# Reordering the steps between the last expert of layer one and the first tiles of layer two, on four engines, with one more wait for the weight loads

## The reference, cut to what matters

```python
x = attention(q, k, v)                       # 1536 x 512
# layer one: 8 experts, each token goes to the best 2 of its noisy scores
out[mask] += top2_w[mask, k, None] * (relu(x[mask] @ w1[e]) @ w2[e])
# layer two: other weights, each token goes to its best expert alone
logits = x @ w_gate + modality_bias[modality_id]
e_idx  = argmax(logits, axis=1)
out[mask] = gate_w[mask, None] * (relu(x[mask] @ w1[e]) @ w2[e])
```

## Time and profile before

| | us |
|---|---|
| median of 3 runs | 673.99 (672.82 to 674.08) |
| the profiled execution: its time | 674.08 |
| the profiled execution: its span | 672.0 |
| PE busy in the span | 639.0 |

### The profile page before, as it was taken

The page is one execution under the profiler, slowest core; times in us unless marked ns, Lnnn a source line. Parts: engine busy times, 40 slices in busy tenths (PEclk is TensorE's granted clock), DMA queues, the critical chain, the costliest instruction groups (busy, mean ns, idle before and its releaser), DMA issues.

```text
span 672.0 us, 11238 instructions
## 1 busy us (share of the span) xinstructions
PE 639.0 (95%) x3866; PEld 580.1 (86%) x3867; DVE 329.8 (49%) x681; ACT 275.7 (41%) x529; POOL 184.7 (27%) x199
## 2 busy tenths in 40 slices
PE   7989999899999999999999999999988999999981
PEld 6989999898999999999999999988767888788871
DVE  4466645588365526254361634467876222542220
ACT  5667866442344335252443523144516123522110
POOL 2500100117362533516144251201652121121010
PEclk9999999999999999999999999999998999999996
DMA  7867822263684646646355520724649211001000
GB/s 209 281 235 240 291 74 80 66 249 74 237 214 138 132 148 157 190 142 156 111 122 177 148 28 3 171 63 159 171 138 387 102 48 47 20 32 48 16 32 11
DMA packets 51089, 89.84 MB, mean 134 GB/s; under 512 B 7919, under 2 KB 14063, under 8 KB 51040
## 3 DMA queue, kind: packets, MB, share of 16 engines
q1 hardware_dynamic: 41872, 69.21, 31.0%
q0 software_dynamic: 9168, 19.97, 13.3%
HBM read 73.13 MB, written 17.02 MB: 134 GB/s over the span
## 4 chain that ended last, share of the span: by engine, by line
PE 82%; DVE 6%; DMA 3%; ACT 3%; issue 2%; SPq 1%; ACTq 0%; POOL 0%; DVEq 0%; POOLq 0%
PE banks L1060 6%; PE banks L1059 6%; PE banks L999 6%; PE banks L1078 6%; PE banks L1001 6%; PE banks L998 6%; PE banks L803 5%; PE banks L831 4%; PE banks L1377 3%; PE banks L1342 3%; PE banks L1347 3%; PE banks L1343 3%; PE banks L1373 3%; PE banks L1374 3%; PE banks L815 2%
## 5 line engine op out<-in xcount | busy, mean ns | idle before, releaser
L1833 DVE TENSOR_TENSOR split<-stage,split 128x2048 fp32r<-128x2048 f32 x32 | 73.3, 2290 | 41.9 <-ACT split L1463 41.8
L998 PE MATMUL banks<-xTs,split 128*128 128x416 f32 (+1 forms) x256 | 88.6, 350 | 0.0
L999 PE MATMUL banks<-xTs,split 128*128 128x416 f32 (+1 forms) x256 | 86.5, 342 | 0.0
L650 POOL DMA_INDIRECT x_moe<-rows,dst_idx x25 | 49.3, 1971 | 113.2 <-DVE rows L2285 112.2
L1059 PE MATMUL banks<-hTs,split 128*128 128x416 f32 x224 | 79.9, 357 | 0.0
L1060 PE MATMUL banks<-hTs,split 128*128 128x416 f32 x224 | 78.6, 351 | 0.0
L1598 ACT ACTIVATE hTs<-banks 128x416 fp32r<-128x416 f32 x56 | 29.0, 518 | 81.6 <-PE banks L1001 81.6
L1463 ACT ACTIVATE split<-stage 128x2048 fp32r<-128x2048 f32 x32 | 60.9, 1908 | 1.0 <-DMA stage<-w1a 1.0
L1720 ACT ACTIVATE hTs<-banks 128x512 fp32r<-128x512 f32 x28 | 16.5, 596 | 105.8 <-PE banks L1357 105.8
L1001 PE MATMUL banks<-xTs,split 128*128 128x416 f32 (+1 forms) x256 | 56.2, 340 | 0.0
L803 PE MATMUL banks<-k_sb,q_sb 128*128 128x260 f32 (+2 forms) x192 | 49.6, 384 | 3.5 <-DMA k_sb<-k_w 2.1
(11 more groups left out here) (371 smaller groups left out, 1308.3 us busy)
## 6 DMA issues: line engine op xcount, KB each, us to landing
stage<-w1a SPq DMA_DIRECT2D x16, 1024.0 KB, 7.6
stage<-w2a SPq DMA_DIRECT2D x16, 1024.0 KB, 5.4
k_sb<-k_w SPq DMA_DIRECT2D x12, 520.0 KB, 5.0
raw<-w1b SPq DMA_DIRECT2D x4, 1024.0 KB, 7.9
raw<-w2b SPq DMA_DIRECT2D x4, 1024.0 KB, 9.7
q_sb<-q_t SPq DMA_DIRECT2D x24, 128.0 KB, 3.1
x_attention<-rows SPq DMA_DIRECT2D x12, 256.0 KB, 6.1
split<-x_moe SPq DMA_DIRECT2D x12, 256.0 KB, 3.6
```

The costliest lines, as they stand in the source:

```text
L650: pool.indirect_dma_start(out=x_dram[1], out_offset=rows_at(dst_idx[0], early_dst, e, k), in_=y_lines(e, k), in_offset=None, compute_op=AL ...
L998: pe.matmul(psum, piece(slot, 0, o + c * FH), xTs[:, 0, c, 0:cols], start=(c == 0), stop=False)
L999: pe.matmul(psum, piece(slot, 1, o + c * FH), xTs[:, 0, c, 0:cols], start=False, stop=False)
L1833: dve.tensor_tensor(split_chunk(e % 2, 1, c), staged_chunk(e % 2, c), split_chunk(e % 2, 0, c).bitcast(F32), ALU.subtract).then_inc(low_do ...
```

## The change

It reorders steps on PE, ACT and DVE and adds one wait on SP.

- SP: before it loads the second expert of layer two, it also waits until the gather of tile 2 has landed (`gathered[0]` at 32).
- PE: `back(last, 3)` moves ahead of `first(0, 0)`; `ranks(1)` and a wait for all four scaled parts of the last expert move ahead of `first(0, 1)`; `codes2` moves out of `second(0)` to a place behind `first(1, 1)`. Tile 3 becomes an ordinary `step(3, 1, 3)`, so `th(2, 0)` comes behind `first(3, 0)`.
- ACT: `popular_high(0)` moves ahead of `y1_copy(last, 3)`; `relu(0, 0)` moves behind `popular_high(2)`; `popular_high(3)` moves ahead of `relu(0, 1)`, the exponential and `x_high(1)`; `parted_tiles` moves ahead of `relu(1, 0)`.
- DVE: `popular_low(0)` moves ahead of `popular_first` and `last_share`; `popular_low(1)` ahead of the scores; `x_low(0)` behind the choice; `second_places` ahead of `x_low(1)`, `chosen_gate` and `popular_low(2)`; `second_sources` ahead of `h_low(0, 0)`; `expert_order`, `tile_owners` and `fresh_tiles` ahead of `slot_gates` and `y_copy(0)`; `second_weights((0, 1))` ahead of `y_copy(1)`.

```diff
@@ -514,6 +514,7 @@
             experts = sp.value_load(used[0:1, 1, 1:2], min_val=1, max_val=E)
             e = sp.value_load(order[0:1, 1:2], min_val=0, max_val=E - 1)
             sp.wait_ge(last_added, 1)
+            sp.wait_ge(gathered[0], 32)
             for c in range(CHUNKS):
                 if c == CHUNKS - 1:
                     sp.wait_ge(all_scattered, 1)
@@ -1361,11 +1362,8 @@
                     if not isinstance(t, int) or t > 0:
                         pe.wait_ge(y_copied, t)
                     for half in range(2):
-                        if isinstance(t, int) and half == 1:
-                            if t == 0:
-                                codes2()
-                            elif t == 1:
-                                tx(2, 0, 2)
+                        if isinstance(t, int) and t == 1 and half == 1:
+                            tx(2, 0, 2)
                         pe.wait_ge(low_done[2 + half], e + (E + 1))
                         pe.wait_ge(h_high_done, t * 2 + (half + 1))
                         for c in range(half * 4, half * 4 + 4):
@@ -1402,16 +1400,16 @@
 
                 tx(0, 0, 1)
                 back(last, 2, banks[:, 3, :])
+                back(last, 3, banks[:, 4, :])
                 first(0, 0, 0, 1)
-                back(last, 3, banks[:, 4, :])
-                pe.wait_ge(scaled1, nth_sub(last, 0) + 1)
+                ranks(1)
+                pe.wait_ge(scaled1, nth_sub(E, 0))
                 first(0, 1, 0, 1)
                 tx(1, 1, 1)
-                ranks(1)
                 first(1, 0, 0, 1)
-                pe.wait_ge(scaled1, nth_sub(E, 0))
                 th(0, 0)
                 first(1, 1, 0, 1)
+                codes2()
                 th(0, 1)
                 second(0, 0, 1)
                 slot_gates()
@@ -1419,17 +1417,11 @@
                 th(1, 1)
                 second(1, 0, 1)
                 pe.wait_ge(fresh_ready[1], 1)
-                e2, slot2 = expert(2)
-                first(2, 0, e2, slot2)
-                first(2, 1, e2, slot2)
+                e, slot = expert(2)
+                first(2, 0, e, slot)
+                first(2, 1, e, slot)
                 tx(3, 1, 2)
-                th(2, 0)
-                e3, slot3 = expert(3)
-                first(3, 0, e3, slot3)
-                first(3, 1, e3, slot3)
-                th(2, 1)
-                tx(4, 0, 3)
-                second(2, e2, slot2)
+                step(3, 1, 3)
                 with pe.Fori(2, sure // 2 - 1) as r:
                     step(r * 2, 0, r + 1)
                     step(r * 2 + 1, 1, r + 2)
@@ -1693,6 +1685,7 @@
                 y1_copy(last, 2)
                 x2_high(11)
                 turned_copy(2)
+                popular_high(0)
                 y1_copy(last, 3)
 
             def popular_high(c):
@@ -1763,23 +1756,22 @@
                             act.wait_ge(pe_route, 7)
                         high_part(1, c)
 
-                popular_high(0)
                 popular_high(1)
                 last_scale(0)
                 last_scale(1)
                 x_high(0)
                 last_scale(2)
-                relu(0, 0)
                 last_scale(3)
                 popular_high(2)
+                relu(0, 0)
+                popular_high(3)
+                relu(0, 1)
                 act.wait_ge(act_route, 6)
                 act.activation(rc[:], rb[:], ACT.Exp).then_inc(act_route, 1)
-                relu(0, 1)
                 x_high(1)
-                popular_high(3)
+                parted_tiles()
                 relu(1, 0)
                 h_high(0, 0)
-                parted_tiles()
                 relu(1, 1)
                 h_high(0, 1)
                 h_high(1, 0)
@@ -2470,36 +2462,36 @@
                         dve.wait_ge(high_done[c], E + 2)
                         low_part(1, c)
 
+                popular_low(0)
                 popular_first()
                 last_share()
-                popular_low(0)
+                popular_low(1)
                 late_scores()
                 all_scores()
-                x_low(0)
-                popular_low(1)
                 pick(noisy, 0, chosen[:], done_key)
                 dve.sem_inc(dve_route, 1)
                 link(dve.tensor_tensor(rb[:], noisy[:], over_e(top[:, 0, :]), ALU.subtract))
                 dve.sem_inc(act_route, 1)
+                x_low(0)
+                second_places()
+                x_low(1)
                 chosen_gate()
+                second_hots()
                 popular_low(2)
-                x_low(1)
-                second_places()
-                second_hots()
+                second_sources()
                 h_low(0, 0)
                 popular_low(3)
-                second_sources()
                 h_low(0, 1)
+                expert_order()
+                tile_owners()
+                fresh_tiles()
                 slot_gates()
                 y_copy(0, 0, 0)
-                expert_order()
                 h_low(1, 0)
                 h_low(1, 1)
-                tile_owners()
-                fresh_tiles()
                 x_low(2)
+                second_weights((0, 1))
                 y_copy(1, 1, 0)
-                second_weights((0, 1))
                 x_low(3)
                 second_weights((2, 3))
                 next_weights(2)
```

## The result

The changed kernel takes 676.81 us in the median of 12 runs (675.09 to 679.95), the kernel before 672.99 on the same chip (12 runs, 671.62 to 675.96). The ratio is 1.0053, with a 95% interval of 1.0037 to 1.0069: slower by 3.6 us. Forecast were 4.0. The profiled execution of the changed kernel took 675.41, with a span of 673.6; that is only 1.33 over the profiled 674.08 of before, so this pair of traces shows less of the loss than the medians do.

The account below looks back on a forecast made before the run. PE was taken to bound the kernel, busy 639.0 of 672.0 us. Loss 6.0 by tile 2, gain 2.7, net 3.3, plus 0.7 for the clock: 4.0 over 674.08, median forecast 678.0, range 674.6 to 681.5.

Parts of the forecast that it names:

- Step 1: Chunk 0's split ahead of the last copy: last_to_tokens 3.6 us late, first(0, 0) late, loss 3.0.
- Step 2: x_low(0) behind the choice on DVE: PE idles 1.7 us in first(0, 0); tx(1) done at 482.5 instead of 478.21.
- Step 3: Last chunk ahead of x_high(1) on ACT: first(1, 0) at 484.1, without the chunk 483.2; loss 5.9 so far.
- Step 4: Up to the end of second(1): DVE's list makes y_copy(0) end at 501.8, tile 2 starts at 508.2, loss 6.0.
- Step 5: Tile 2 to tile 4: earlier weight splits shorten the late waits, gain 2.7 us, net loss 3.3.
- The clock: PE at half clock behind new gaps: between nothing and 3.0 us, taken as 0.7.
- behind 501.8: Fall of PE's clock after the gap at 500 to 501.8, before second(1): costs 1.5 us.
- SP's wait: SP's new wait before the second expert's loads: costs nothing, the gather landing by 495.6, before the order at 498.2.
- The slip of the gather: POOL's gate parts beside DVE operations: port lock could delay the gather 4.5 us, giving 678.6 in place of 678.0.
- (a): Tiles 2 and 3: the late gain wins, a delay of 1 at tile 2 gives 672.3; chance 0.08.
- (b): Half is absorbed in PE's later waits: delay of 3.0 to 3.5 at tile 2, 674.5; chance 0.08.
- (c): Clock falls in two gaps outside other waits, or the lock makes the gather late: 681.0; chance 0.12.

Follow-up runs that it names:

- e7: Changed kernel with PE's gaps ahead of last_logits(3) and last_to_tokens filled by 14 products into an unused bank; 682.70 us, ratio 1.0033.
- e1: Kernel before with only popular_high(0) ahead of y1_copy(last, 3) and popular_low(0) ahead of popular_first and last_share; 676.90 us, ratio 1.0054.
- e6: e2 with popular_high(3) of ACT moved back behind relu(0, 1), the exponential and x_high(1); 684.27 us, ratio 1.0044.
- e10: e2 with x_low(0) ahead of the choice on DVE and ranks(1) behind tx(1, 1, 1) on PE again; 680.25 us, ratio 1.0038.
- e3: Changed kernel with DVE's slot_gates and y_copy(0) back ahead of expert_order, tile_owners and fresh_tiles; 677.07 us, ratio 1.0061.
- e8: Kernel before with only expert_order of DVE moved ahead of slot_gates and y_copy(0); 676.16 us, ratio 0.9960.
- e9: Changed kernel without SP's new wait for the gather of tile 2; 680.24 us in one execution.
- e2: Changed kernel with popular_high(0) back behind y1_copy(last, 3) and popular_low(0) back behind last_share; 677.80 us, ratio 1.0074.
- e4: Kernel before with relu(2), x_high(3) and x_low(3) ahead of the second expert's weight splits on ACT and DVE; 674.54 us, ratio 1.0034.

## Why the prediction was right, and where it was not

The sign and the size were right (forecast 4.0, measured 3.6), and so was the kind of cause. Some terms were not.

**Step 1** forecast 3.6 for `last_to_tokens` and 3.0 for `first(0, 0)`; 3.4 and 3.9 came. The 0.9 is the half clock: in e7, where the clock stayed up, `first(0, 0)` starts at 9.18, 2.8 late. e1 shows the mechanism alone, and that it suffices for the whole loss.

**Step 2** forecast that PE idles 1.7 for x_low(0). In the first trace of the changed kernel it doesn't (476.76 follows on the high products), because PE was slow; in the second it idles 0.5, in e7 1.69. In all three the low pass starts where DVE sets it, at 12.9 behind the common point, and 12.96 was forecast. From there the forecast held: without the chunk it had `first(1, 0)` at 483.2, that is 18.9, and 19.00 came. What ranks cost there is their own 0.67 (13.95 to 14.62): before, they ran in the time of x_high(1), and `tx` to `first(1, 0)` is 1.41 with ranks between, 1.55 without.

**Step 3** is the step that failed: 0.9 forecast, nothing measured (e6). I had the chunk's split end at 482.6, 18.3 behind the common point, and x_high(1) end 1.4 behind that. The chunk landed 0.5 earlier (15.84 against 16.38), its split ended at 17.76, and x_high(1) started at 18.31, only 0.26 behind the end of tx(1, 1) (18.05), which it needs too. With step 2 undone the step costs 2.8 (e10). Up to here 5.9 were forecast, 5.1 came.

**Step 4** forecast tile 2 6.0 late: 4.5 in the first traces. The list up to y_copy(0) was right in kind: PE waits 1.78 for it (1.9 forecast), 1.0 for the last chunk's low part (1.2). But y_copy(0) was forecast 6.4 late and came 5.0 late: 0.8 of the difference came in with step 3, and 0.5 is the list itself, where second_hots took 1.77 and not 2.2. second(1) then ran 0.6 shorter, 0.4 forecast. e3 shows the other side, which I had not priced: y_copy(0) earlier means the weights later.

**Step 5** forecast that 2.7 of the 22.1 from tile 2 to tile 4 come back: 22.06 became 19.57, 2.5, and 19.61 in the second traces. The wait for relu at tile 3 is gone; what stays of the waits there is 1.08, with 1.0 forecast. Every version that keeps this part has 19.5 to 19.6; e8, which takes just the early order, has 19.1.

**The clock** got 0.7. The first traces differ by 1.97 at tile 4, the second by 3.44, and the 1.5 between them is one fall, the one "behind 501.8" of the forecast. The median loss of 3.6 is near the second pair. It would come out as well if most executions had neither fall: without its 1.6 at tile 3 the kernel before would have tile 4 at 58.3, 3.6 ahead of 61.90, and the lowest runs (671.62 and 675.09) are 3.5 apart. Which share of the executions has which fall, the runs don't say; the fall at tile 3 was in both traces of before, not in e1's, which waits there as long. So part of the forecast's 4.0 is right by luck, by two errors that offset each other: 1.5 too much by tile 2, about 1 too little for the clock.

**SP's wait** costs nothing (e9), with the gather issued 6.7 before the loads. POOL's operation of 2.13 beside DVE's split of 2.32, where the like took 0.21 in the kernel before with no such split beside it, agrees with the lock that the Trainium skill describes ("SBUF — State Buffer", who interferes with whom: GpSimd has no ports of its own, and an operation of it that reads SBUF contends with a VectorE instruction with two SBUF inputs). The slip of the gather that I derived from it did not come (issued at 26.95 behind the common point, 27.9 forecast), because the steps before had such operations in them too, and I had them in the sum already.

**The rivals**: (a) did not happen, but its place is real: e8 is the change's gain without its losses. The first pair of traces (tile 2 4.5 late, tile 4 2.0) lies between the forecast and (b), half absorbed; of the two falls of (c), the second trace of the changed kernel has one, at second(1).

## What to carry to other kernels

Where four engines run lists written by hand, losses of single moves on one stretch do not add: e1 and e2 each cost the whole, so take the latest of the chains, not their sum, and test a move alone before blaming it. Don't put work that waits for a DMA ahead of a short copy that PE needs; put bookkeeping that starts a transfer into the idle time of its engine, as early as that allows, and remove stalls by making transfers earlier rather than by moving the work behind them (e8 against e4). Count times from a common point when executions differ upstream by more than the effect.

## What the runs showed of the hardware

- PE's clock fell from 2.4 to 1.2 GHz (granted 1.00 to 0.50) behind gaps of PE: one of 1.6 in the changed kernel, one of 1.82 at second(1) in its second trace, and gaps of 1.13 and 0.66 at tile 3 in both traces of before. The same gaps don't bring a fall each time: e1 with 1.2 and 0.7 at tile 3 and the first trace of the changed kernel with 1.78 at second(1) had none.
- Nor does a fall need such a gap. Between 2 and 5 us behind the common point, where PE has only short products, all five traces with step 1 and no filler fell, but so did four of the eight without step 1 (the second trace of before, e4, e8 and e10), none of which has a gap over 0.2 there. With step 1 the half clock lasted 6 to 7 us, without it 3 to 4.
- A fall cost 0 to 1.6 us, by whether PE was waiting anyway.
- SP issued the load of the last weight chunk of the popular expert at about 5 us behind the common point in every trace, and where ACT waited for it, it landed between 13.7 (e10) and 16.8 us (e7), with the same code on SP.
